# Attention and two feed-forward layers on one core: the order of a head pair's steps on four engines is changed

## The reference, cut to what matters

```python
def _attn_ref(q, k, v):                       # (4, 8, 576, 64)
    q_d, k_d, v_d = means of 4 tokens
    out_d = softmax(q_d @ k_d.T / 8) @ v_d    # 144 pooled tokens
    out_up = np.repeat(out_d, 4, axis=2)
    scores = where(abs(i - j) < 4, q @ k.T / 8, -1e9)
    out_local = softmax(scores) @ v
    return out_up + out_local

def reference(...):
    x = attn_out.transpose(0, 2, 1, 3).reshape(2304, 512)
    h = x @ w_in;  x = (h * sigmoid(h)) @ w_out                # 512 -> 2048 -> 512
    h = x @ w_in2; return (h * sigmoid(1.702 * h)) @ w_out2
```

## Time and profile before

| what | us |
|---|---|
| median of 3 runs (808.3 to 808.89) | 808.36 |
| the profiled execution's own time | 809.36 |
| its span | 807.6 |
| TensorE busy | 794.6 |
| VectorE busy | 643.2 |
| ScalarE busy | 533.1 |
| GpSimd busy | 198.2 |

### The profile page before, as it was taken

One profiled execution on the slowest core, in us unless ns is written; L12 is line 12 of the kernel. 1 busy time (PEld: TensorE's weight loads), 2 busy tenths in 40 slices (PEclk: granted clock), 3 DMA queues, 4 the chain that ended last, 5 costly groups with the idle time before them and its releaser, 6 DMA issues.

```text
span 807.6 us, 15746 instructions
## 1 busy us (share of the span) xinstructions
PE 794.6 (98%) x5864; PEld 763.7 (95%) x5864; DVE 643.2 (80%) x899; ACT 533.1 (66%) x849; POOL 198.2 (25%) x217
## 2 busy tenths in 40 slices
PE   9999899999999999999999999999999999999998
PEld 5666599999999999999999999999999999999998
DVE  6999889999998678998678898899565688456466
ACT  5888865677655678555687556678456786465673
POOL 4799866620175320445100000000000000000000
PEclk9999999999999999999999999999999999999999
DMA  8887647787877887688977778868987778878773
GB/s 274 279 248 247 186 135 271 260 297 225 273 246 255 276 307 250 219 243 267 293 267 250 238 252 259 262 220 275 304 279 249 277 253 265 300 252 266 270 259 132
DMA packets 100571, 205.51 MB, mean 254 GB/s; under 512 B 8592, under 2 KB 56208, under 8 KB 100496
## 3 DMA queue, kind: packets, MB, share of 16 engines
q1 hardware_dynamic: 100496, 204.51, 77.0%
HBM read 160.96 MB, written 43.52 MB: 253 GB/s over the span
## 4 chain that ended last, share of the span: by engine, by line
PE 88%; DVE 8%; ACT 2%; issue 1%; POOL 0%; DVEq 0%; POOLq 0%; ACTq 0%
PE hid L356 43%; PE yp L382 42%; DVE sums L1195 2%; DVE pband L1205 1%; DVE mxb L1202 1%; DVE smb L1216 1%; DVE x L1237 1%; ACT pband L1132 1%; PE yp L398 1%; ACT pavg L1147 0%; DVE wh L320 0%; PE sc L1391 0%; PE pt L1267 0%; ACT pta L1123 0%; DVE rca L1227 0%
## 5 line engine op out<-in xcount | busy, mean ns | idle before, releaser
L356 PE MATMUL hid<-xs,wh 128*128 128x384 f32 x2016 | 351.3, 334 | 0.8 <-issue 0.6
L356 PEld LDWEIGHTS hid<-xs,wh 128*128 128x128 f32 x2016 | 349.4, 188 | 1.9 <-issue 1.6
L382 PE MATMUL yp<-gr,wh 128*128 128x384 f32 x1968 | 342.2, 334 | 0.0
L382 PEld LDWEIGHTS yp<-gr,wh 128*128 128x128 f32 x1968 | 341.1, 188 | 0.2
L311 ACT ACTIVATE wh<-wr 128x1024 fp32r<-128x1024 f32 (+1 forms) x164 | 164.7, 1005 | 150.1 <-PE hid L356 122.4
L574 DVE TENSOR_TENSOR gr<-G,gr 128x768 fp32r<-128x768 f32 x144 | 138.8, 971 | 52.5 <-ACT gr L454 52.5
L454 ACT ACTIVATE gr<-G 128x768 fp32r<-128x768 f32 x144 | 121.8, 846 | 67.8 <-PE yp L382 67.8
L320 DVE TENSOR_TENSOR wh<-wr,wh 128x1024 fp32r<-128x1024 f32 x76 | 95.2, 1252 | 19.0 <-ACT wh L311 18.8
L417 ACT ACTIVATE G<-G 128x1152 f32<-128x1152 f32 x48 | 55.7, 1160 | 0.2 <-DVE G L569 0.2
L538 DVE TENSOR_TENSOR hv<-p,hid 128x384 f32<-128x384 f32 x48 | 26.4, 549 | 30.7 <-PE hid L356 29.5
L564 DVE TENSOR_TENSOR G<-hv,hid 128x384 f32<-128x384 f32 x48 | 26.4, 550 | 28.0 <-PE hid L356 28.0
(11 more groups left out here) (105 smaller groups left out, 742.2 us busy)
## 6 DMA issues: line engine op xcount, KB each, us to landing
wh<-rests SPq DMA_DIRECT2D x72, 512.0 KB, 3.9
wr<-sums_out SPq DMA_DIRECT2D x48, 512.0 KB, 4.8
wr<-in_w_out SPq DMA_DIRECT2D x36, 512.0 KB, 5.4
rests<-wh SPq DMA_DIRECT2D x36, 512.0 KB, 3.6
wr<-sums_in SPq DMA_DIRECT2D x40, 384.0 KB, 4.0
wr<-in_w_in SPq DMA_DIRECT2D x40, 256.0 KB, 3.7
qk<-in_qkT SPq DMA_DIRECT2D x11, 576.0 KB, 4.9
G<-in_w_in SPq DMA_DIRECT2D x12, 512.0 KB, 5.2
```

The source lines that it names most:

```text
L356: last = eng.matmul(hid[:, at, 0:HALF], lhsT=wh[:, w % SLOTS, part, a % 4, cc * P:(cc + 1) * P], rhs=xs[:, rest, q, cc, :], start=start an ...
L382: last = eng.matmul(yp[:, at + m, 0:HALF], lhsT=wh[:, w % SLOTS, part, p % 4, m * P:(m + 1) * P], rhs=gr[:, p, rest, :], start=start and p ...
```

## The change

It does five things.

1. TensorE: unit n+1's `band_scores` are issued before unit n-1's `avg_product`, right behind the mask.
2. ScalarE: unit n's `nga` and pooled exponentials come before the two `pta` copies of unit n-1; `normalise` comes before the copy of the pooled result in every unit.
3. VectorE: unit n-2 is added to `x` in body n behind the subtraction (before: unit n-1, at the end of body n), and the next unit's `sums` come last in the body.
4. Rests: weight batch 0's moves from VectorE (unit 4) to GpSimd in two halves (units 3 and 13), T2's from VectorE (unit 14) to GpSimd in two chunks (unit 14).
5. The sums of the first layer's weight pair 6 move from GpSimd's units 13 and 14 to the end of its unit 15, next to pair 7's, and the loads of the weights wait for the load before them and no longer for GpSimd's sums.

```diff
@@ scalar body
+                    eng.wait_ge(a_max, u.n + 1)
+                    eng.activation(nga[:], mxa[:], ACT.Copy, scale=-scale_avg).then_inc(a_neg, 1)
...
                 if not first:
                     for j in range(NLG, NG):
                         group(old, j)
...
-                if last is not None and u.n == 0:
+                else:
                     normalise(u)
@@ vector body
+                    if u.n > 1:
+                        add_results(u.before().before())
                     eng.wait_ge(avg_sc, u.n + 1)
                     eng.tensor_reduce(mxa[:], ...
...
-                    if not last:
-                        sums(u.after())
...
                     eng.reciprocal(rca[:], rca[:]).then_inc(a_rcp, 1)
+                    if not last:
+                        sums(u.after())
@@ tensor body
                 band_product(old)
-                    if last is not None and not last:
-                        band_mask(u.after())
-                    avg_product(old)
+                if last is False:
+                    band_mask(u.after())
+                    band_scores(u.after())
+                avg_product(old)
@@ tables
-    RESTS = {14: T2}
-    RESTS_W = {4: 0}
+    LAST_RESTS = {14: T2}
+    HALF_RESTS = {3: 0, 13: 1}
@@ gpsimd sum_weights
+                    for p in range(PAIRS - 2, PAIRS):
+                        sum_first(p)
+                        sum_second(p)
+                elif u.n <= 2 * (PAIRS - 2):
@@ sync body
-                        eng.wait_ge(ffn.w0_sum, 4 * u.half - 2)
+                        eng.wait_ge(ffn.w0_in, DMA_INC * u.half)
```

More of the change, by code:

```diff
@@ L1071, in body @@
                     ffn.rest_x(eng, 0, *POOL_RESTS[u.n])
+                if u.n in HALF_RESTS:
+                    ffn.rest_weights(eng, 0, HALF_RESTS[u.n])
+                if u.n in LAST_RESTS:
+                    for chunk in range(2):
+                        ffn.rest_x(eng, 0, LAST_RESTS[u.n], chunk)
                 if not first:
@@ L1149, in body @@
                                        accum_out=sma[:, c, 0:1]).then_inc(a_exp, 1)
-                if last is not None and u.n == 0:
+                if not first:
+                    for j in range(NLG, NG):
+                        group(old, j)
+                if last is None:
+                    eng.wait_ge(v_sum, summed(UNITS - 1))
+                    ffn.scalar(eng, True)
+                else:
                     normalise(u)
@@ L1211, in body @@
                                       AX.X, ALU.max).then_inc(a_max, 1)
-                if not first:
-                    early(u.n)
-                if last is not None:
+                if last is None:
+                    add_results(u.before().before())
+                    rests()
+                    add_results(u.before())
+                else:
                     eng.wait_ge(b_exp, u.n + 1)
@@ L1229, in body, with rests @@
                     eng.reciprocal(rca[:], rca[:]).then_inc(a_rcp, 1)
[L1230 to L1255, removed]
+                    if not last:
+                        sums(u.after())
+            def rests():
+                eng.wait_ge(ffn.w_lo, 1)
+                ffn.rest_weights(eng, 1)
+                eng.wait_ge(ffn.x_lo, 5)
+                ffn.rest_x(eng, 0, B22)
+                ffn.rest_x(eng, 0, T4)
+                ffn.rest_weights(eng, 2)
+                ffn.vector(eng, True)
             eng.memset(zeros[:], 0.0).then_inc(zero, 1)
@@ L1363, in body @@
                     ffn.tensor(eng, True)
-                else:
-                    if first:
-                        band_mask(u)
+                if first:
+                    band_mask(u)
                     band_scores(u)
[L1368 to L1373, removed]
                     avg_scores(u)
-                if first:
                     keep_warm(IDLE[0], pt)
@@ L1378, in body @@
                     band_mask(u.after())
-                if not first:
-                    for j in range(NLG, NG):
-                        group(old, j)
-                    band_product(old)
-                    if last is not None and not last:
-                        band_mask(u.after())
-                    avg_product(old)
+                    band_scores(u.after())
+                    return
+                if u.n == 1:
+                    keep_warm(IDLE[1], pt)
+                for j in range(NLG):
+                    group(old, j)
+                if last is not None:
+                    avg_scores(u)
+                for j in range(NLG, NG):
+                    group(old, j)
+                band_product(old)
+                if last is False:
+                    band_mask(u.after())
+                    band_scores(u.after())
+                avg_product(old)
             def keep_warm(times, to):
```

56 lines of the change are left out of this document (29 added, 27 removed).

## The result

| | before | changed |
|---|---|---|
| median, us | 808.69 (5 runs, 808.3 to 810.04) | 812.99 (5 runs, 811.75 to 813.09) |
| profiled execution | 809.36 | 811.75 |
| its span | 807.6 | 809.9 |

The account below looks back on a forecast made before the run. TensorE sets the second stage's time, with attention's VectorE-ScalarE ring ahead of it. Terms +0.1, +1.8, -1.8, -1.0, +1.15 gave +0.25 on 809.36: 809.6 profiled, 808.6 us median, range 806.8 to 810.8.

Parts of the forecast that it names:

- price of 0 for GpSimd's four added sums: Opening of the products: GpSimd's added sums beside VectorE's rests cost 0 us, as TensorE is full there.
- the range: Whole kernel's median: 806.8 to 810.8 us, around the forecast of 808.6.
- The ring, 5.97 a unit: Attention: one chain of VectorE and ScalarE links, from `rca` through `mxa` and `nga` to `rca`, lasting 5.97 us per unit.
- predicted +0.25 for the whole of attention: Up to the first products: sum of first units, ring, unit 14, unit 15 and pooled product, 0.25 us later than before.
- stated bounds (5.87 to 6.07): Attention: uncertainty of the new ring's length per unit in us, -1.3 to +1.3 us over 13 units.
- Unit 14, -1.8: Attention: with T2's rest off VectorE, unit 14 falls from 7.79 to 5.97 us, saving 1.8.
- The pooled product ahead of the products, 1.15: End of attention: unit 14's `avg_product` waits for both `pta` copies, so first products start 1.15 us after `rca`.
- the bound of 1.6 that I had given from another mechanism: Opening of the products: at most 1.6 us if VectorE's rests and GpSimd's added sums block one another at SBUF.
- Rival 2, the lower clock: Opening: TensorE's gap in unit 15 makes first products run at half speed, 1.7 us more, 810.3; chance 0.17.
- Rivals 1 and 3: Attention: ring not closing, 806.0 us, chance 0.13; late addition a second ring, 811.2, chance 0.10 shared with opening's contention.
- The step from 809.6 to 808.6: Whole kernel: profiled forecast 809.6 us lowered to a median of 808.6, the profiled execution lying 1.0 above the median.

Follow-up runs that it names:

- e5: Changed kernel plus six matmuls of zeros ahead of the last averages' products, filling TensorE's gap: 811.98 us, ratio 1.0031.
- e6: Changed kernel plus the six matmuls of zeros, with pair 7's sums behind the first two pairs of output-weight sums: 809.86 us, ratio 1.0005.
- e10: Kernel before with only parts 4 and 5 of the change, plus four matmuls of zeros ahead of the first products: 806.16 us, ratio 0.9966.
- e1: Changed kernel with pair 7's four GpSimd sums moved behind the first two pairs of output-weight sums, gap not filled: 813.33 us, ratio 1.0047.
- e9: Kernel before plus four matmuls of zeros ahead of its first products, nothing else changed: 809.14 us, ratio 1.0003.
- e2: Changed kernel with pair 6's four sums put back into GpSimd's units 13 and 14: 810.21 us, ratio 1.0011.
- e3: Kernel before with only parts 4 and 5 of the change, no matmuls of zeros: 807.3 us, ratio 0.9974.
- e8: Kernel before with parts 4 and 5, pair 7's sums late and four matmuls of zeros ahead of the first products: 805.89 us, ratio 0.9954.
- e12: Changed kernel plus the six matmuls of zeros and four more GpSimd sums of the weights' shape: 817.35 us, ratio 1.0095.

## Why the prediction failed

The step that failed is the price of 0 for GpSimd's four added sums, on the ground that TensorE is full above them; measured at full clock they cost 2.1 us. e5, without any stretch at half clock, still took 811.98, outside the range; e6, with the sums' queue relieved as well, took 809.86, inside it. By steps of the prediction:

- **The ring, 5.97 a unit.** Right in its mechanism, each link within 0.03, the sum 0.06 short: 6.03. The excess is 0.03 in `sums` (1.25, not 1.22) and 0.01 in each of three others. Over 13 units, with 0.15 in the first two, it is +0.9 on a predicted +0.25 for the whole of attention, and 1.22 was measured. It lay within the stated bounds (5.87 to 6.07).
- **Unit 14, -1.8.** Right: the unit is as long as the others, and e10 shows it also in the old order (5.82).
- **The pooled product ahead of the products, 1.15.** Right: 101.55 - 100.38 = 1.17, then 6.28 to the long run, predicted 6.25.
- **"GpSimd does four more sums, under products in which TensorE is full": priced at 0. This is the step that failed.** I asked only whether TensorE waits for the sums' own results. Behind them on GpSimd stand the output-weight sums, behind those SyncE's stores and loads, and behind these batch 16, which TensorE needs some 53 us after the start of the long run. Measured 2.1 us (e5 to e6), above the bound of 1.6 that I had given from another mechanism. The eight sums took GpSimd from 107.06 to 114.04, 6.98 us, where 8 x 0.73 is 5.84; one took 1.46 while VectorE did a rest.
- **Rival 2, the lower clock, 0.17 for 1.7 us.** It does happen, and oftener than its chance said: the gap was 1.46 long, the clock fell in 3 of 5 executions of the changed kernel and in 6 of 7 of e1, and in e1's profile the stretch cost 2.95, not 1.7. What it holds of the changed kernel's 4.3 is not shown. Filling the gap took the excess over before from 4.3 to 2.8, but the intervals of the two ratios overlap (1.0032 to 1.0054 and 1.0021 to 1.0042), and the five executions do not order by their clock.
- **Rivals 1 and 3.** The ring closed, so the first fell. TensorE did wait for the late addition, 6.8 us in 13 waits, 0.7 at most, but that wait lay beside the ring: `mxb` never waited for scores.
- **The step from 809.6 to 808.6.** It was taken because the profiled execution lay 1.0 above the median of three runs. The later groups of before, 17 to 30 runs, have medians of 809.04 to 809.33, so most of that 1.0 was the luck of three runs, and the forecast was too low by it. From 809.6 the longer attention (1.22 - 0.25 = 0.97) and the queue (2.1) give an estimate of 812.7; 812.99 was measured, and 811.98 with the gap filled.

How queue and clock stand together: with the gap filled, relieving the queue gains 2.1 (e5 to e6). Without, it gains 0.3 of the excess over before (changed to e1, 4.3 to 4.0), which the scatter covers. With the queue relieved, filling the gap gains 3.3 (e1 to e6); with the queue as the change has it, 1.5 at most. Neither order gives the clock a share of its own, and whether the two costs add is not shown: 2.1 and 0.3 differ by less than the intervals allow. e1's wait of 4.56 us speaks for one hiding a part of the other. What is left without either, 0.7 in e6, holds the 1.2 us of a longer attention, less what before pays for its own stretches at half clock; the split of those two is not measured, since e9 did not remove them. Parts 1 to 3 together lose: from e10 to e5 it is 5.7 us, of which 4.3 are attention (long run behind the first `mxb`: 96.79 and 101.05); behind it TensorE waits 2.5 us in e5 and 0.5 in e10 (together 6.3, a little more than was measured). Parts 4 and 5 win 2.0 without and 2.9 with the filling, two values whose intervals overlap.

## What to carry to other kernels

When work is added to an engine that nobody waits for, follow its queue to the first transfer it releases, and that transfer's queue to the next load: what counts is how much time that load has in hand, not who is idle now. A gap of TensorE just ahead of a full stretch has a second price, which comes in some executions only; so a single profile may not show it, and filling the gap with matmuls of zeros is cheap where they stand in the gap itself. Do not add two such costs unseen: a stretch at half clock also gives a queue time, so each is to be tried with and without the other. And where two moves each take one thing out of a ring, add up the new ring first: here `sums` and `mxa` came in with 1.9 us for 1.7 of exponential and copies that left.

## What the hardware showed that was not expected

- With nearly the same gap (1.46 us in the changed kernel's profile, 1.47 in e1's) the clock stayed at 1.00 in one execution and fell to 0.50 for 6.8 us in the other. Both kernels also have executions of the other kind. The Trainium skill, "TensorE: Matmul & The Clock Gate", Part 1, says that the number of slow matmuls at the start of a kernel changes from run to run; the rows show the like in the middle of one, and here the gap alone does not decide it (1.44 in e2, never in 11 executions). Stretches came in lengths of 3.4 and 6.8 us.
- Matmuls of zeros that stand behind the gap of 2.46 us did nothing (e9, 11 of 12 executions with a stretch). Where that gap is gone and the same number fills the next one, of 1.08 us in e3, there was no stretch left (e10 and e8, 11 executions).
- One GpSimd sum of 128x256 takes 0.73 us alone and 1.46 when VectorE's rest of two SBUF operands (110.32 to 111.64) is running; VectorE's rest of 128x1024 takes 1.22 alone and 1.71 across two GpSimd sums:

```profile
105.76 1.22 DVE L321 TENSOR_TENSOR wh<-G,wh 128x1024 fp32r<-128x1024 f32 x1
...
110.32 1.32 DVE L321 TENSOR_TENSOR wh<-G,wh 128x768 fp32r<-128x768 f32 x1 [0.46 <-ACT wh L311]
...
113.45 1.71 DVE L321 TENSOR_TENSOR wh<-G,wh 128x1024 fp32r<-128x1024 f32 x1 [0.33 <-ACT wh L311]
```

  The Trainium skill, "SBUF — State Buffer", section "SBUF: two separate sides", says that the two engines lock one another out for a whole instruction in such a pair. The rows agree in kind, and either engine can be the one that pays: in the kernel before, the last of these three rests took 1.23, and the GpSimd sum that started in the same moment, at 113.35, took 1.82. In e12, four more sums delayed the output-weight sums by (121.15 - 108.85) - (114.51 - 108.30) = 6.1 us, counted from the long run's start, instead of some 3; half of it was made up further down the queue (batch 16 went out 49.6 - 46.4 = 3.2 later).
